# Attention and two MLP layers on one core: TensorE kept at work with zeros, and VectorE, GpSimd and ScalarE reordered in the attention stage

## The chip, the cores and the metric

The kernel runs on one core of a Trainium2 chip. The metric is the device time of one execution in microseconds (us), as the median of several runs. Engines: TensorE (PE) does matrix products, VectorE (DVE) and ScalarE (ACT) elementwise work and can read PSUM, GpSimd (POOL) elementwise work on SBUF, SyncE (SP) issues the loads.

## The reference

```
scores = q @ k^T / 8            # (4 batches, 8 heads, 576 x 576), head_dim 64
thresh = max(scores) - tau      # tau = 0.02
scores = where(scores >= thresh, scores, -1e9)
attn   = exp(scores - max) / (sum + 1e-9)
x      = attn @ v               # as (2304 tokens, 512)
h = x @ w_in;  g = s * relu(h)**2 + b;        x = g @ w_out       # d_ff 2048
h = x @ w_in2; g = h * sigmoid(1.702 * h);    out = g @ w_out2
```

## The kernel before

All products but those of the probabilities are done in three parts: an operand is split in a high part (`_hi`, rounded for the fast fp32r mode) and a low part (`_lo`, the rest), and hi x hi, hi x lo and lo x hi are added up. For scores the three parts take two products, because q and its low part lie above each other on the partitions (`q_hl`). High parts are made by ScalarE, low parts by VectorE or GpSimd.

Attention goes by tiles: 128 (or 96) queries of one head against 576 keys. Two tiles make a beat; there are 160 tiles, and 85 beats with the last pieces. Each engine has its own order, written out by hand as a loop over beats, and semaphores join them:

- TensorE: scores of the beat's two tiles into two PSUM buffers (`scores_of`; `buffer_free` waits until `mask` is through with the buffer's last tile), then for the first 32 tiles the transposes of the probabilities of tile j - 4 (`turn_tile`), then a context product, probabilities times v (`context_of`), whose result is called a piece. In beats 3 to 14 the piece is alone: 128 tokens of a pair of heads into the one PSUM bank `shared`. From beat 16 on pieces ride: 192 tokens, beside the scores in PSUM. From beat 15 on each beat also does one step of the first MLP layer (`hidden`, and `output` three steps later), s = beat - 15.
- VectorE: `row_max` (scales the scores in PSUM and takes the row maximum, through an accumulator that is read by a small instruction of its own), `limit_of` (maximum and tau), `mask` (drops exponentials under the limit and adds up the row), `invert_pair`, `context_lo` (low part of a piece, `act_lo`), `gated` and `gated_lo` (the MLP's gate and its low part `g_lo`), and from tile 32 on `turn` (32x32 transposes, in place of TensorE's).
- ScalarE: `exponent`, `context_hi` (high part of a piece, `act_hi`), `copy_main` and `copy_tails` (transposed probabilities out of PSUM), the high parts of q, k and the weight slabs.
- GpSimd: low parts of q, k (`splits`) and the slabs, `norm` (probabilities times the inverse sum), `add_eps_pair`.
- SP: loads, in order.

A piece that is alone has one bank, so the product waits for the low part of the piece before; its waits at the beat are, in order, for the copies of the transposed probabilities and then:

```
                    if piece > 0:
                        pe.wait_ge(context_lo_ready, piece)
                i = VALUE_OF[piece]
                pe.wait_ge(v_loaded[i % 2], 16 * (i // 2 + 1))
```

The first step of the MLP waits for all twelve such pieces (`context_lo_ready, LONE_PIECES`). After the attention come the rest of the first layer and then the second layer, which is done in pairs of token tiles and slabs with seven products in place of eight. Neither is touched.

Of the kernel before, what the change touches and what calls it, by code (L numbers as in the profile page):

```python
# [233 lines left out]
SPLITS_BEHIND = PE_TILES // 2 + 2  # L234

HASTY = 3 * PAIRS_PER_BATCH - 1

# [114 lines left out]
def build(nc, q, k, v, consts_in, ident_in, slabs, twin_in, twin_out, out):  # L354
    ctx = ExitStack()
    with ctx:
# [3 lines left out]
        def sbuf(stack, name, shape, dt=F32):  # L360
            return stack.enter_context(nc.sbuf_tensor(name, shape, dt))
# [74 lines left out]
        row_sum_eps = sbuf(attn, "row_sum_eps", [P, STATS])  # L436
        row_inv = sbuf(attn, "row_inv", [P, STATS])
        eps_pair = sbuf(attn, "eps_pair", [P, 2])
        attn.close()

        b_hi.insert(0, sbuf(ctx, "b_hi0", [P, PRODUCT_COUNT, 2, TOK], F32R))
# [23 lines left out]
        consts_ready = sem("consts_ready")  # L465
        lower_set = sem("lower_set")
        pads_zeroed = sem("pads_zeroed")
        table_loaded = sem("table_loaded")
        q_loaded = [sem(f"q_loaded{n}") for n in range(Q_RING)]
        k_loaded = [sem(f"k_loaded{n}") for n in range(2)]  # L470
# [139 lines left out]
        def _(sp):  # L610
# [50 lines left out]

            load_k(0)
            load_q(0)
            sp.dma_start(consts[:, 0:3], consts_in).then_inc(consts_loaded, 16)
            load_k(1)
            load_q(1)
            sp.dma_start(ident[:], ident_in).then_inc(ident_loaded, 16)
            load_q(2)
# [60 lines left out]
        def _(pe):  # L729
# [232 lines left out]
            def mlp(s):  # L962
# [4 lines left out]
                if 0 <= s < STEPS:  # L967
                    hidden(s)

            for beat in range(BEATS):  # L970
                due = turn_due(beat - MLP_FROM)
                for j in tiles_of(beat):
                    if j < TILES or (j % 2 == 0 and due is not None) or (j % 2 == 1 and riding(beat) is not None):
                        buffer_free(j)
                    if j % 2 == 0 and due is not None:
                        turn_riding(*due)
                    if j % 2 == 1 and riding(beat) is not None:
                        context_of(riding(beat))
                    if j < TILES:
                        scores_of(j)  # L980
                    if 0 <= j - 4 < PE_TILES:
                        turn_tile(j - 4)
                if alone(beat) is not None:
                    context_of(alone(beat))
                mlp(beat - MLP_FROM)
# [16 lines left out]

        @block.vector
        def _(dve):
            nc.vector.memset(lower_c[0:64, :], 0.0).then_inc(lower_set, 1)
            nc.vector.memset(lower_c[64:128, :], 1.0).then_inc(lower_set, 1)
            dve.wait_ge(consts_loaded, 16)
            nc.vector.tensor_scalar(scale_c, tau_in, 0.0, -SCALE, ALU.is_ge, ALU.mult).then_inc(consts_ready, 1)
            nc.vector.tensor_scalar(tau_c, tau_in, 0.0, None, ALU.max).then_inc(consts_ready, 1)
            dve.wait_ge(k_hi_ready, 1)  # L1010
            nc.vector.tensor_tensor(k_lo[key_slot(0)][:], k_raw[key_slot(0)][:], k_hi[key_slot(0)][:].bitcast(F32),
                                    ALU.subtract).then_inc(k_lo_ready, 1)
            dve.wait_ge(q_hi_ready, 1)
            nc.vector.tensor_tensor(q_hl[0][:, 0:q_width(0)], q_raw[:, 0, 0:q_width(0)],
                                    q_hl[0][:, 0:q_width(0)].bitcast(F32), ALU.subtract
                                    ).then_inc(q_lo_ready, 1)
            dve.wait_ge(consts_ready, 2)

            def row_max(j):
# [6 lines left out]
                                        accum_out=neg_max[0:m, j % STATS:j % STATS + 1]  # L1026
                                        ).then_inc(max_ready, 1)

            def limit_of(j):
                m, r = rows_of(j), j % STATS  # L1030
                dve.wait_ge(max_ready, j + 1)
                nc.vector.tensor_scalar(limit[0:m, r:r + 1], neg_max[0:m, r:r + 1], tau_c[0:m, :], None, ALU.add  # L1032
                                        ).then_inc(limit_ready, 1)

            def invert_pair(j):
# [5 lines left out]
            def mask(j):  # L1041

                m, r = rows_of(j), j % STATS
                dve.wait_ge(limit_ready, j + 1)
                dve.wait_ge(exp_ready, j + 1)
                if j % 2 == 1 and riding(j // 2) is not None:
                    dve.wait_ge(context_hi_ready, riding(j // 2) + 1)
                if j % 2 == 0 and turn_due(j // 2 - MLP_FROM) is not None:
                    dve.wait_ge(x_ready, turns_by(j // 2 - MLP_FROM))
                p = prob[0:m, j % PROBS, :].rearrange("p (a n) -> p a n", a=2)  # L1050
                nc.vector.scalar_tensor_tensor(  # L1051
                    out=p, in0=scores[j % 2][0:m, :, 0:HALF], scalar=limit[0:m, r:r + 1],
                    in1=p, op0=ALU.is_le, op1=ALU.mult,
                    accum_out=row_sum[0:m, r:r + 1]).then_inc(masked, 1)
# [101 lines left out]
            def low_block(d, i):  # L1156
# [2 lines left out]
                nc.vector.tensor_tensor(g2_lo[:, i, :], gate2[:, i % 2, :], g2_hi[:, i, :].bitcast(F32),  # L1159
                                        ALU.subtract).then_inc(g2_lo_ready, 1)  # L1160

            for beat in range(BEATS):
                s = beat - MLP_FROM
                for j in tiles_of(beat):
                    if j < TILES:
                        row_max(j)
                        limit_of(j)
                    if j % 2 == 0 and alone(beat - 1) is not None:
                        context_lo(alone(beat - 1))
                    if j % 2 == 0 and 0 <= j - 2 < TILES:  # L1170
                        invert_pair(j - 2)
                    if j % 2 == 0 and s >= 1:
                        gated(s - 1)
                for j in tiles_of(beat):
                    if j < TILES:
                        mask(j)
                    if j % 2 == 0 and s >= 2:
                        gated_lo(s - 2)
                if riding(beat) is not None:
                    context_lo(riding(beat))  # L1180
                for j in tiles_of(beat, 2):
                    if PE_TILES <= j < TILES:
                        turn(j)
# [39 lines left out]
        def _(act_eng):  # L1223
# [180 lines left out]
            for beat in range(BEATS):  # L1404
                s = beat - MLP_FROM
                if alone(beat - 1) is not None:
                    context_hi(alone(beat - 1))
                for j in tiles_of(beat):
                    if j < TILES:
                        exponent(j)  # L1410
                    if j % 2 == 0 and 0 <= j - 4 < PE_TILES:
                        copy_tails(j - 4)
                    if j % 2 == 0 and turn_due(s) is not None:
                        x_riding(s)
                for j in tiles_of(beat, 4):
                    if 0 <= j < PE_TILES:
                        copy_main(j)
                if riding(beat) is not None:
                    context_hi(riding(beat))
                if tile_ends(s - 1) and s + 1 < STEPS:  # L1420
                    slab_in_hi(s + 1)
                if s >= 1:
                    gated_hi(s - 1)
                if tile_ends(s):
                    copy_rows(s - OUT_LAG)
                    if s < STEPS:
                        gate_of(s)
                if s >= 1:
                    slab_out_hi(s - 1)
                for i in range(2, len(Q_LOADS)):  # L1430
                    if q_split_beat(i) == beat:
                        split_q(i)
                for e in range(2, HEADS):
                    if key_split_beat(e) == beat:
                        split_k(e)
                if not tile_ends(s):
                    if 0 <= s < STEPS:
                        gate_of(s)
                    if 0 <= s + 2 < STEPS:
                        slab_in_hi(s + 2)  # L1440
# [58 lines left out]
        def _(pool):  # L1499
# [14 lines left out]
            def split_k(e):  # L1514

                pool.wait_ge(k_hi_ready, e + 1)
                if e == 1:
                    pool.wait_ge(k_lo_ready, 1)
                nc.gpsimd.tensor_tensor(k_lo[key_slot(e)][:], k_raw[key_slot(e)][:], k_hi[key_slot(e)][:].bitcast(F32),
                                        ALU.subtract).then_inc(k_lo_ready, 1)  # L1520

# [25 lines left out]
                                        wout_hi[n % OUT_HI][:].bitcast(F32), ALU.subtract  # L1547
                                        ).then_inc(wout_lo_ready, 1)

            def splits(beat):  # L1550
                for i in range(2, len(Q_LOADS)):
                    if q_split_beat(i) + 1 == beat:
                        split_q(i)
                for e in range(2, HEADS):
                    if key_split_beat(e) + 1 == beat:
                        split_k(e)

            pool.wait_ge(pads_zeroed, 2)
            split_k(1)
            split_q(1)  # L1560
            for beat in range(BEATS):
                s = beat - MLP_FROM
                if s >= 2:
                    slab_out_lo(s - 2)
                if beat < SPLITS_BEHIND:
                    splits(beat)
                for j in tiles_of(beat, 2):
                    if 0 <= j < TILES:
                        norm(j)
                if s >= 2:  # L1570
                    pool.wait_ge(g_lo_ready, s - 1)
                if beat >= SPLITS_BEHIND:
# [105 lines left out]
```

## Time and profile before

| | |
|---|---|
| median of 3 runs | 1013.93 us (1013.07 to 1015.03) |
| profiled execution | 1013.14 us |
| its span | 1011.3 us |
| PE busy | 988.5 us (98%) |
| DVE busy | 796.9 us (79%) |
| ACT busy | 606.3 us (60%) |
| POOL busy | 658.3 us (65%) |

The span runs from the first to the last instruction; the execution's own time has 1.84 us more around it. Matmul ends are modelled, so that PE's busy share says little about its rate; where PE stands idle and what ended the wait is to be read from the timeline and the waits. Attention ends near 484 us.

### The profile page before, as it was taken

To read this page: it belongs to the slowest core of one execution; us is meant where nothing else is said; L and a number is where in the kernel's file an instruction comes from. 1 tells how busy PE (TensorE), PEld (TensorE's weight loads), DVE (VectorE), ACT (ScalarE), POOL (GpSimd) and SP (SyncE) were. 2 spreads that over 40 slices of the span, in tenths; PEclk is the share of its full clock that TensorE was granted. 3 is DMA by queue.
4 is the path that set the end of the run, shared out by engine and by line. 5 is a ranking of instruction groups with operands and counts; after the bars stand their busy time and mean duration, and the time that the engine had idled before them with its cause. 6 is when DMAs were issued, how large, how long until landed. Compare 5 with 4: busy or idle time off the path is not lost.

```text
span 1011.3 us, 18111 instructions
## 1 busy us (share of the span) xinstructions
PE 988.5 (98%) x5872; PEld 890.6 (88%) x5872; DVE 796.9 (79%) x1747; ACT 606.3 (60%) x1124; POOL 658.3 (65%) x714
## 2 busy tenths in 40 slices
PE   5999999999999999999999999999999999999998
PEld 4888888888888888888899999998898989898897
DVE  6999999999999999999646765877667777556663
ACT  5887666666576666665545756554546545454453
POOL 5768997778888788887657775444534544445442
PEclk9999999999999999999999999999999999999999
DMA  6235776788777888678733441112122321222212
GB/s 205 82 99 168 204 207 208 193 242 237 211 192 196 225 218 222 191 185 214 207 122 126 172 162 34 41 64 84 42 84 71 118 84 43 83 82 106 84 47 78
DMA packets 97580, 142.48 MB, mean 141 GB/s; under 512 B 10320, under 2 KB 68944, under 8 KB 97488
## 3 DMA queue, kind: packets, MB, share of 16 engines
q1 hardware_dynamic: 97488, 141.34, 47.8%
q8 instruction: 48, 0.79, 0.3%
q14 instruction: 44, 0.36, 0.1%
HBM read 102.96 MB, written 4.72 MB: 106 GB/s over the span
## 4 chain that ended last, share of the span: by engine, by line
PE 87%; DVE 10%; issue 1%; ACT 1%; DMA 0%; POOL 0%; SPq 0%; DVEq 0%; POOLq 0%; ACTq 0%
PE shared L825 12%; PE y_ps L844 11%; PE shared L918 10%; PE y_ps L942 10%; PE scores L942 10%; PE scores L918 8%; PE scores L739 8%; PE scores L801 7%; PE scores L825 5%; PE y_ps L864 5%; DVE scores L1025 4%; DVE prob L1051 3%; PE scores L864 2%; DVE blocks L1065 1%; DVE limit L1032 1%
## 5 line engine op out<-in xcount | busy, mean ns | idle before, releaser
L1248 ACT ACTIVATE prob<-scores,neg_max 128x576 f32<-128x576 f32 (+1 forms) x160 | 118.6, 741 | 126.1 <-DVE scores L1025 124.0
L1590 POOL TENSOR_TENSOR a_sum_lo<-a_sum,a_hi 128x256 fp32r<-128x256 f32 x96 | 70.1, 740 | 182.7 <-DVE scores L1147 124.0
L1025 DVE TENSOR_SCALAR_CACHE_REDUCE scores<-scores,consts 128x576 f32<-128x576 f32 (+1 forms) x160 | 129.5, 809 | 18.1 <-PE scores L739 16.6
L1539 POOL TENSOR_TENSOR w_lo<-w_raw,win_hi 128x512 fp32r<-128x512 f32 x96 | 129.0, 1344 | 22.1 <-ACT win_hi L1290 17.7
L1546 POOL TENSOR_TENSOR w_lo<-w_raw,wout_hi 128x512 fp32r<-128x512 f32 x96 | 126.4, 1316 | 23.6 <-ACT wout_hi L1297 23.5
L1533 POOL TENSOR_SCALAR prob<-prob,row_inv 128x576 f32<-128x576 f32 (+1 forms) x160 | 126.5, 803 | 5.5 <-DVE row_inv L1039 5.0
L1051 DVE SCALAR_TENSOR_TENSOR prob<-scores,limit,prob 128x576 f32<-128x576 f32 (+1 forms) x160 | 128.1, 808 | 0.9 <-ACT act_hi L1258 0.9
L825 PE MATMUL shared<-act_hi,win_hi 128*128 128x384 f32 x280 | 94.9, 339 | 1.1 <-DVE gate L1081 0.9
L825 PE MATMUL shared<-act_hi,w_lo 128*128 128x384 f32 x280 | 94.4, 337 | 0.0
L739 PE MATMUL scores<-k_hi,q_hl 128*128 128x288 f32 (+1 forms) x320 | 78.0, 326 | 16.8 <-DVE prob L1051 9.0
L825 PE MATMUL shared<-act_lo,win_hi 128*128 128x384 f32 x280 | 94.0, 336 | 0.0
L1088 DVE SCALAR_TENSOR_TENSOR g_lo<-gate,consts,g_hi 128x384 fp32r<-128x384 f32 x96 | 92.6, 964 | 0.2 <-ACT g_hi L1311 0.2
L1065 DVE STREAM_TRANSPOSE blocks<-prob 128x576 f32<-128x576 f32 (+1 forms) x128 | 91.4, 751 | 1.3 <-DMA prob_t<-blocks 1.1
L1159 DVE TENSOR_TENSOR g_lo<-gate,g_hi 128x384 fp32r<-128x384 f32 x96 | 62.2, 650 | 33.4 <-ACT g_hi L1382 32.8
L1311 ACT ACTIVATE g_hi<-gate,consts 128x384 fp32r<-128x384 f32 x96 | 59.0, 615 | 38.8 <-PE y_ps L864 28.0
L1374 ACT ACTIVATE gate<-scores 128x384 f32<-128x384 f32 x48 | 23.6, 491 | 94.9 <-DVE scores L1147 94.9
L1382 ACT CAST g_hi<-gate 128x384 fp32r<-128x384 f32 x96 | 49.2, 515 | 49.4 <-DVE gate L1154 40.0
L739 PEld LDWEIGHTS scores<-k_hi,q_hl 128*128 128x128 f32 (+1 forms) x320 | 49.9, 183 | 32.3 <-DVE prob L1051 14.3
L844 PE MATMUL y_ps<-wout_hi,g_hi 128*128 128x512 f32 x192 | 75.6, 394 | 0.0
L844 PE MATMUL y_ps<-wout_hi,g_lo 128*128 128x512 f32 x192 | 75.5, 393 | 0.0
L801 PE MATMUL scores<-prob_t,v_sb 128*64 128x192 f32 x800 | 73.9, 331 | 1.2 <-DVE prob L1051 0.9
L844 PE MATMUL y_ps<-w_lo,g_hi 128*128 128x512 f32 x192 | 74.9, 390 | 0.0
(154 smaller groups left out, 2945.1 us busy)
## 6 DMA issues: line engine op xcount, KB each, us to landing
w_raw<-slabs SPq DMA_DIRECT2D x93, 512.0 KB, 4.1
a_raw<-twin_in SPq DMA_DIRECT2D x24, 512.0 KB, 4.5
o_raw<-twin_out SPq DMA_DIRECT2D x24, 512.0 KB, 3.5
prob_t<-blocks SPq DMA_DIRECT2D x96, 120.0 KB, 2.7
k_raw<-k SPq DMA_DIRECT2D x32, 288.0 KB, 4.2
prob_t<-blocks SPq DMA_DIRECT2D x96, 96.0 KB, 2.9
v_sb<-v SPq DMA_DIRECT2D x26, 320.0 KB, 4.3
q_raw<-q SPq DMA_DIRECT2D x40, 192.0 KB, 4.4
```

What stands on the lines that cost most here:

```text
L739: mm = nc.tensor.matmul(scores[j % 2][0:m, half, 0:HALF], q_hl[i % Q_RING][:, q0:q0 + m], part[key_slot(e)][:, half * HALF:(half + 1) * HALF],
L801: mm = nc.tensor.matmul(place, v_sb[:, i % 2, side, c, :], rows, start=(c == 0), stop=(c == KEY_CHUNKS - 1))
L825: mm = nc.tensor.matmul(bank[:, 0:TOK], wp[:, w], act_at(xp, c, tile * TOK, TOK), start=(c == 0 and k == 0), stop=(c == DC - 1 and k == 2))
L844: mm = nc.tensor.matmul(y_ps[g][:], gp[:, n % 2, toks], wp[:, :], start=(f == 0 and k == 0), stop=(f == SLABS - 1 and k == 2))
L918: mm = nc.tensor.matmul(twin_bank(x), wp, xp, start=(c == 0 and k == 0), stop=(c == 1 and k == 2))
L942: mm = nc.tensor.matmul(z_bank(tile, g), gp[:, i, toks], wp, start=(e == 0 and i < 2 and k == 0), stop=(e == TWIN_SLABS - 1 and i >= 2 and ...
L1025: nc.vector.tensor_scalar(place, place, scale_c[0:m, :], None, ALU.mult, ALU.min, accum_out=neg_max[0:m, j % STATS:j % STATS + 1]).then_in ...
L1051: nc.vector.scalar_tensor_tensor(out=p, in0=scores[j % 2][0:m, :, 0:HALF], scalar=limit[0:m, r:r + 1], in1=p, op0=ALU.is_le, op1=ALU.mult, ...
L1248: nc.scalar.activation(prob[0:m, j % PROBS, :].rearrange("p (a n) -> p a n", a=2), scores[j % 2][0:m, :, 0:HALF], ACT.Exp, bias=neg_max[0: ...
L1533: nc.gpsimd.tensor_scalar(prob[0:m, j % PROBS, :], prob[0:m, j % PROBS, :], row_inv[0:m, r:r + 1], 1.0, ALU.mult, ALU.mult).then_inc(norme ...
L1539: nc.gpsimd.tensor_tensor(in_of(w_lo, n), in_of(w_raw, n), win_hi[n % IN_HI][:].bitcast(F32), ALU.subtract).then_inc(win_lo_ready, 1)
L1546: nc.gpsimd.tensor_tensor(out_of(w_lo, n), out_of(w_raw, n), wout_hi[n % OUT_HI][:].bitcast(F32), ALU.subtract).then_inc(wout_lo_ready, 1)
```

## The change

Five edits. The order of TensorE gets products of zeros that nobody reads: ten ahead of the first scores, eight behind the scores of tile 1, seven behind those of tile 3, into the unused columns of a PSUM bank. VectorE does head 1's low part instead of GpSimd, and its constants after the first low parts; SP loads head 1's keys ahead of the constants. VectorE takes the limits of a beat's two tiles in one operation, behind `context_lo` and `gated_lo`, which now stand ahead of both masks. ScalarE does `context_hi` of a riding piece ahead of `copy_main`. GpSimd, in beat 1, splits only load 2 ahead of the norms and the rest behind them.

```diff
+AWAKE_FIRST = 10
+AWAKE = (0, 8, 0, 7)
...
+        zeros = sbuf(attn, "zeros", [P, P])
...
             load_q(0)
+            load_k(1)
             sp.dma_start(consts[:, 0:3], consts_in).then_inc(consts_loaded, 16)
-            load_k(1)
...
+            def keep_awake(n):
+                for _ in range(n):
+                    nc.tensor.matmul(y_ps[2][:, 2 * P:3 * P], zeros[:], zeros[:], start=True, stop=True)
+
+            pe.wait_ge(zeros_set, 1)
+            keep_awake(AWAKE_FIRST)
...
                     if j < TILES:
                         scores_of(j)
+                    if j < len(AWAKE):
+                        keep_awake(AWAKE[j])
...
         def _(dve):
+            nc.vector.memset(zeros[:], 0.0).then_inc(zeros_set, 1)
...
-            dve.wait_ge(consts_loaded, 16)
-            nc.vector.tensor_scalar(scale_c, tau_in, 0.0, -SCALE, ALU.is_ge, ALU.mult).then_inc(consts_ready, 1)
-            nc.vector.tensor_scalar(tau_c, tau_in, 0.0, None, ALU.max).then_inc(consts_ready, 1)
...
+            split_k(0)
             dve.wait_ge(q_hi_ready, 1)
...
+            dve.wait_ge(consts_loaded, 16)
+            nc.vector.tensor_scalar(scale_c, tau_in, 0.0, -SCALE, ALU.is_ge, ALU.mult).then_inc(consts_ready, 1)
+            nc.vector.tensor_scalar(tau_c, tau_in, 0.0, None, ALU.max).then_inc(consts_ready, 1)
             dve.wait_ge(consts_ready, 2)
...
+                dve.wait_ge(max_ready, j + 2)
+                nc.vector.tensor_scalar(limit[0:m, r:r + 2], neg_max[0:m, r:r + 2], tau_c[0:m, :], None, ALU.add
                                         ).then_inc(limit_ready, 1)
...
+            split_k(1)
             for beat in range(BEATS):
                 s = beat - MLP_FROM
                 for j in tiles_of(beat):
                     if j < TILES:
                         row_max(j)
-                        limit_of(j)
-                    if j % 2 == 0 and alone(beat - 1) is not None:
-                        context_lo(alone(beat - 1))
                     if j % 2 == 0 and 0 <= j - 2 < TILES:
                         invert_pair(j - 2)
                     if j % 2 == 0 and s >= 1:
                         gated(s - 1)
+                if alone(beat - 1) is not None:
+                    context_lo(alone(beat - 1))
+                if s >= 2:
+                    gated_lo(s - 2)
+                if 2 * beat < TILES:
+                    limit_pair(2 * beat)
                 for j in tiles_of(beat):
                     if j < TILES:
                         mask(j)
-                    if j % 2 == 0 and s >= 2:
-                        gated_lo(s - 2)
...
+                if riding(beat) is not None:
+                    context_hi(riding(beat))
                 for j in tiles_of(beat, 4):
                     if 0 <= j < PE_TILES:
                         copy_main(j)
-                if riding(beat) is not None:
-                    context_hi(riding(beat))
...
-            split_k(1)
             split_q(1)
...
-                if beat < SPLITS_BEHIND:
+                if beat == 1:
+                    split_q(2)
+                elif beat < SPLITS_BEHIND:
                     splits(beat)
                 for j in tiles_of(beat, 2):
                     if 0 <= j < TILES:
                         norm(j)
+                if beat == 1:
+                    splits(beat, 3)
```

## Rows read from the trace of the kernel before

**Rows 1.** Page, the chain that ended last, by engine.
```profile
PE 87%; DVE 10%; issue 1%; ACT 1%; DMA 0%; POOL 0%; SPq 0%; DVEq 0%; POOLq 0%; ACTq 0%
```
**Rows 2.** Busy time by window: PE, PEld, DVE, ACT, POOL, clock, DMA share, GB/s.
```profile
150.00:200.00 50.00, 49.81 (x317) 43.62 (x314) 47.77 (x122) 32.15 (x60) 36.70 (x44) 1.00 0.73 199
```
**Rows 3.** Timeline, 0 to 22 us: start, duration, instruction, idle before and releaser.
```profile
4.58 0.15 DVE L1008 TENSOR_SCALAR consts<-consts 128x1 f32<-128x1 f32 x1 [3.62 <-DMA consts<-consts_in]
...
5.84 0.85 PE L739 MATMUL scores<-k_hi,q_hl 128*128 128x288 f32 x2 [5.84 <-DVE q_hl L1014]
6.00 0.67 ACT L1238 CAST k_hi<-k_raw 128x576 fp32r<-128x576 f32 x1 [1.26 <-DMA k_raw<-k]
...
6.82 1.40 POOL L1519 TENSOR_TENSOR k_lo<-k_raw,k_hi 128x576 fp32r<-128x576 f32 x1 [4.50 <-ACT k_hi L1238]
...
8.36 0.82 PE L739 MATMUL scores<-k_hi,q_hl 128*128 128x288 f32 x2 [1.18 <-POOL k_lo L1519]
...
11.62 0.85 PE L739 MATMUL scores<-k_hi,q_hl 128*128 128x288 f32 x2 [1.96 <-DVE prob L1051]
...
16.00 0.85 PE L739 MATMUL scores<-k_hi,q_hl 128*128 128x288 f32 x2 [2.10 <-DVE prob L1051]
...
21.32 0.53 PE L739 MATMUL scores<-k_hi,q_hl 128*128 128x288 f32 x2 [1.32 <-DVE prob L1051]
```
**Rows 4.** Timeline, one beat of the stage with attention alone.
```profile
29.23 0.53 PE L739 MATMUL scores<-k_hi,q_hl 128*128 128x288 f32 x2 [0.32 <-DVE prob L1051]
...
30.67 0.42 PE L739 MATMUL scores<-k_lo,q_hl 128*128 128x288 f32 x2
...
31.11 0.28 DVE L1073 TENSOR_TENSOR act_lo<-shared,act_hi 128x128 fp32r<-128x128 f32 x1
...
31.38 0.81 DVE L1025 TENSOR_SCALAR_CACHE_REDUCE scores<-scores,consts 128x576 f32<-128x576 f32 x1
...
31.64 1.31 PE L801 MATMUL shared<-prob_t,v_sb 128*64 128x128 f32 x20
...
32.10 0.14 DVE L1025 DVE_READ_ACCUMULATOR scores<-scores,consts 128x1 f32 x1
...
32.41 0.81 DVE L1051 SCALAR_TENSOR_TENSOR prob<-scores,limit,prob 128x576 f32<-128x576 f32 x1
...
33.28 0.53 PE L739 MATMUL scores<-k_hi,q_hl 128*128 128x288 f32 x2 [0.33 <-DVE prob L1051]
```
**Rows 5.** Timeline, 68 to 77 us: context products, and the first MLP product.
```profile
68.10 1.31 PE L801 MATMUL shared<-early_t,v_sb 128*64 128x128 f32 x20 [0.33 <-DVE act_lo L1073]
...
69.73 0.50 PE L739 MATMUL scores<-k_hi,q_hl 128*96 128x288 f32 x2 [0.32 <-DVE prob L1051]
...
71.98 0.19 PEld L825 LDWEIGHTS shared<-act_hi,win_hi 128*128 128x128 f32 x1 [0.34 <-POOL w_lo L1539]
...
75.21 1.84 PE L801 MATMUL scores<-prob_t,v_sb 128*64 128x192 f32 x20
...
76.98 0.51 PE L739 MATMUL scores<-k_hi,q_hl 128*96 128x288 f32 x2
```
**Rows 6.** Waits of PE, 75 to 125 us (total, times, longest); beat 16's timeline.
```profile
PE shared L825 <- DVE gate L1081: 0.9, 3, 0.5
PE scores L801 <- DVE prob L1051: 0.9, 2, 0.5
PE scores L739 <- DVE act_lo L1073: 0.5, 1, 0.5
...
79.35 0.84 ACT L1269 COPY prob_t<-y_ps 128x384 f32<-128x384 f32 x2
...
80.53 0.81 DVE L1051 SCALAR_TENSOR_TENSOR prob<-scores,limit,prob 96x576 f32<-96x576 f32 x1 [0.88 <-ACT act_hi L1258]
```
**Rows 7.** Timeline near 97 us; groups of 150 to 480 us (busy, mean ns).
```profile
96.64 2.09 POOL L1533 TENSOR_SCALAR prob<-prob,row_inv 96x576 f32<-96x576 f32 x2
...
97.17 0.94 DVE L1088 SCALAR_TENSOR_TENSOR g_lo<-gate,consts,g_hi 128x384 fp32r<-128x384 f32 x1
...
L1088 DVE SCALAR_TENSOR_TENSOR g_lo<-gate,consts,g_hi 128x384 fp32r<-128x384 f32 x51 | 34.8, 682 | 0.0
```

More of the change, by code:

```diff
@@ L467, in build @@
         pads_zeroed = sem("pads_zeroed")
+        zeros_set = sem("zeros_set")
         table_loaded = sem("table_loaded")
@@ L1004, in _, with split_k @@
         def _(dve):
+            nc.vector.memset(zeros[:], 0.0).then_inc(zeros_set, 1)
             nc.vector.memset(lower_c[0:64, :], 0.0).then_inc(lower_set, 1)
             nc.vector.memset(lower_c[64:128, :], 1.0).then_inc(lower_set, 1)
-            dve.wait_ge(consts_loaded, 16)
-            nc.vector.tensor_scalar(scale_c, tau_in, 0.0, -SCALE, ALU.is_ge, ALU.mult).then_inc(consts_ready, 1)
-            nc.vector.tensor_scalar(tau_c, tau_in, 0.0, None, ALU.max).then_inc(consts_ready, 1)
-            dve.wait_ge(k_hi_ready, 1)
-            nc.vector.tensor_tensor(k_lo[key_slot(0)][:], k_raw[key_slot(0)][:], k_hi[key_slot(0)][:].bitcast(F32),
-                                    ALU.subtract).then_inc(k_lo_ready, 1)
+            def split_k(e):
+                dve.wait_ge(k_hi_ready, e + 1)
+                nc.vector.tensor_tensor(k_lo[key_slot(e)][:], k_raw[key_slot(e)][:], k_hi[key_slot(e)][:].bitcast(F32),
+                                        ALU.subtract).then_inc(k_lo_ready, 1)
+            split_k(0)
             dve.wait_ge(q_hi_ready, 1)
@@ L1027, in row_max, with limit_pair @@
                                         ).then_inc(max_ready, 1)
-            def limit_of(j):
+            def limit_pair(j):
                 m, r = rows_of(j), j % STATS
-                dve.wait_ge(max_ready, j + 1)
-                nc.vector.tensor_scalar(limit[0:m, r:r + 1], neg_max[0:m, r:r + 1], tau_c[0:m, :], None, ALU.add
+                dve.wait_ge(max_ready, j + 2)
+                nc.vector.tensor_scalar(limit[0:m, r:r + 2], neg_max[0:m, r:r + 2], tau_c[0:m, :], None, ALU.add
                                         ).then_inc(limit_ready, 1)
@@ L1043, in mask @@
                 m, r = rows_of(j), j % STATS
-                dve.wait_ge(limit_ready, j + 1)
+                dve.wait_ge(limit_ready, j // 2 + 1)
                 dve.wait_ge(exp_ready, j + 1)
@@ L1516, in split_k @@
                 pool.wait_ge(k_hi_ready, e + 1)
-                if e == 1:
-                    pool.wait_ge(k_lo_ready, 1)
+                if e == 2:
+                    pool.wait_ge(k_lo_ready, 2)
                 nc.gpsimd.tensor_tensor(k_lo[key_slot(e)][:], k_raw[key_slot(e)][:], k_hi[key_slot(e)][:].bitcast(F32),
@@ L1548, in slab_out_lo, with splits @@
                                         ).then_inc(wout_lo_ready, 1)
-            def splits(beat):
-                for i in range(2, len(Q_LOADS)):
+            def splits(beat, first=2):
+                for i in range(first, len(Q_LOADS)):
                     if q_split_beat(i) + 1 == beat:
```

## The prediction

> **What bounds the kernel now.** I read the chain that ended last first [rows 1]: TensorE has 87% of it, VectorE 10%. The 50 us windows of the middle [rows 2] show where each has its share: there TensorE is busy all the time at a granted clock of 1.00, and VectorE 47.77 of 50 us, so TensorE bounds it and VectorE is close behind. From there to the end TensorE waits for nothing of size, so the time is decided before about 112 us: whatever the changed kernel has won or lost by then arrives at the end as it is. Next I read the timeline of the first 22 us [rows 3], one beat in the stage with attention alone [rows 4], the moments where the context product or the first MLP step waits [rows 5], and TensorE's waits from 75 to 125 us [rows 6].
>
> The start is a chain of single waits: the first score matmul begins at 5.84, the second head's at 8.36 (after GpSimd's k_lo, 6.82 plus 1.40), tile 2 at 11.62, tile 4 at 16.00, tile 6 at 21.32. A pair of 128x288 matmuls takes 0.85 us up to 16.00 and 0.53 at 21.32 [rows 3], so that TensorE runs at its lower level of 1.2 GHz until it has worked nearly without a break from 16.00 on. The clock column says 1.00 in both, so I go by durations.
>
> In the stage with attention alone a beat of two tiles takes 33.28 - 29.23 = 4.05 us [rows 4], and its last link is VectorE's first mask (start 32.41, then 0.87 to the next scores).
>
> **The change, part by part.** Times are against the profiled execution (1013.14 us, span 1011.3 and 1.84 around it); the median shown, 1013.93, is 0.8 higher.
>
> *Start, beats 0 to 2.* VectorE no longer waits 3.62 us for the constants before k_lo. k_hi(0) ends near 4.34, so k_lo(0) runs 4.4 to 5.05, q_lo to 5.5, and scores start at 5.55 instead of 5.84. The key load of head 1 is issued one place (0.48 us) earlier; its conversion, which had waited for the load until 6.00, starts near 5.7 and ends at 6.4. The constants come behind it on SP's queue, near 6.0, which two operations of 0.15 us after q_lo absorb. Then VectorE does k_lo(1) 6.45 to 7.2, at 0.75 for what GpSimd did in 1.40. Its first row maximum starts right behind, 7.1 against 7.32, so it lies in nobody's way, and scores(1) can start at 7.25 instead of 8.36.
> The zeros: one fp32 matmul of 128 columns. The nearest rows are the context products, five slots (two halves side by side) of 128 columns in 1.31 us [rows 4] and of 192 in 1.84 [rows 5]: 0.53/(5 x 64) = 1.66 ns a column, 0.21 to 0.26 us for 128, twice that at the lower clock. The memset is one small operation (GpSimd's 64x768 took 0.73; 0.1 to 0.3 here). So ten zeros run from about 1 us to 5.3 (half of them fast) or 6.0 (all slow). Bounds: nothing, or 0.5 us of delay to scores(0), of which VectorE's k_lo(1) hides most. I take 0. If TensorE is fast by 7 us, scores(1) ends at 8.05, its row maximum at 9.0, the common limit at 9.05, mask(0) starts at 9.2, and scores(2) start at 10.05: 1.55 gained. The eight zeros behind scores(1) take 8 x 0.25 = 2.0 and end at 10.05 as well, so they cost nothing, with no margin. Beat 1 took 4.38; two score groups at the faster pair time (0.3 us less a pair, one group in the chain: 0.5) and one limit (0.13 plus the gap before it) less make 3.65; seven zeros end 0.4 before the next scores. Beat 2 took 5.32 with slow transposes in its chain; I work out 4.1: scores 0.8, row maximum, a wait of about 0.4 for the inverse, row maximum, 1.0 to the mask, 0.87. That wait is new: GpSimd now does norm(0) and norm(1) before the splits of load 3 and head 2 (0.73 + 1.40), and the addition of eps, on which VectorE's next reciprocal waits, stands behind them. Gain at tile 6: 1.55 + 0.73 + 1.22 = 3.5, and 3.4 a beat later, since GpSimd's norm(2) is 0.2 late. Bounds 2.4 to 4.3.
>
> *Beats 4 to 14.* Here the change adds a wait. The context product of a beat waits for act_lo of the piece before (one bank), and act_lo moves from ahead of the second row maximum to behind it. Queued behind the product on TensorE are the next beat's scores. Before, act_lo ends at 31.39 and the product starts at 31.64, 0.25 later [rows 4]; at 68.10 TensorE even waited for act_lo by name, 0.33 us [rows 5]. So it was on the edge already. Now, counted from a beat's first scores: second scores end at 30.67 + 0.42 - 29.23 = 1.86, row maximum from 1.90, its accumulator read at 2.62 (0.72 later, as 31.38 to 32.10), act_lo 2.68 to 2.96, product from 3.21. How soon the next scores can follow: the 192-column product began at 75.21 and scores at 76.98, 1.77 against a duration of 1.84, so 0.07 less than the duration; for 128 columns 1.31 - 0.07 = 1.24. Next beat: 3.21 + 1.24 = 4.45, or 4.42 with the weight load's lead; I take 4.43. The mask path, which loses a limit of 0.13, would allow 3.95, 0.10 under today. So each beat is 0.38 longer: eleven beats, +4.2. Bounds: act_lo could start with the accumulator read (4.37) or 0.17 after it (4.54), the order in which it waits for other things adding nothing: +3.4 to +5.2.
>
> *Beat 15.* The first MLP product needs act_lo of the last piece. Today it starts at 71.98, 2.25 after the beat's scores at 69.73 (they follow the product of 68.10 by 1.63), released by GpSimd. With act_lo ending at 2.8 it starts near 3.0: +0.75 (0.4 to 0.9).
>
> *75 to 112 us.* TensorE's waits there, 0.9 + 0.9 + 0.5 = 2.3 us [rows 6], are the most that this stage can give. At beat 16 the mask at 80.53 had waited 0.88 for the conversion of the piece, which ScalarE did behind two copies from 79.35 (0.84); "piece first" starts that mask near 79.7, 0.83 earlier, and frees 1.0 of TensorE's waits. What moves behind the piece is a copy that the transposes need a beat later; nothing waits. For the rest VectorE must be faster. It loses a limit of 0.13 and two gaps, 0.34 a beat together, but g_lo now runs before both masks. Today g_lo takes 0.61 alone and 0.94 at 97.17, under GpSimd's two norms, which took 2.09 instead of 1.47 [rows 7]: one blocked the other. The new place of g_lo is 1.4 us after the reciprocal that releases the norms, and the norms last 1.47 plus 0.25 of start: a block of about 0.3 in most beats, where the middle of the kernel now has 0.682 - 0.61 = 0.07 on average. So VectorE gains next to nothing a beat. I take -1.4 of the 2.3 (bounds -0.8 and -2.0).
> The Trainium skill states the same as a rule ("SBUF — State Buffer", Who interferes with whom): a VectorE operation with two SBUF inputs and a GpSimd operation that reads SBUF hold one port pair in turn, and the later one waits for the whole of the other. By it g_lo's block would be the rest of the running norm, up to a whole one, 0.75 on GpSimd, not a share of both; the 0.94 here agrees. It speaks against this move, and is the third rival below.
>
> Sum: -3.4 + 4.2 + 0.75 - 1.4 = +0.15 us, so 1013.3 in the terms of the profiled execution and about 1014.0 as a median. No change that can be told: a measurement of this kernel tells 0.2%, 2 us.
>
> **The rivals.**
> *The act_lo wait stays hidden.* Then beats 4 to 14 gain the 0.10 of the limit each (-1.1), beat 15 costs nothing, and the sum is -3.4 - 1.1 - 1.4 = -5.9: 1008.0. For it: the product usually starts just as the transposes end, so today's start does not prove a wait. Against it: 68.10, and in my working the order leaves act_lo no place before 2.6.
> *The zeros run slow.* If zeros don't raise the clock before scores(1), these end at 8.6, eight zeros last 8 x 0.5 = 4.0, and tile 2 starts at 12.6 instead of 11.62. Compared with my 10.05 that is 2.5 us: 1016.5, slower than before. If the seven of beat 1 are slow too, tile 4 starts at 18.4 and the loss is 4.6: 1018.6. It decides as soon as a zero costs over 0.3 us at 8 us. For it: nothing in the trace shows what zeros do to the clock. Against: the rise came about 3 us after the work that began at 16.00, and ten zeros are over 4 us of unbroken work.
> *g_lo against the norms makes VectorE the bound.* VectorE has 50 - 47.77 = 2.2 us in 50 to spare, 0.28 a beat of 6.3 us. With 0.34 won, it is decided from a block of 0.62 a beat on. At 0.70 it costs 0.08 in each of 66 beats, 5 us: 1019. Against: the norms are through, or nearly, when g_lo starts.
>
> **How the numbers follow.** Forecast 0.66, own range 1011.8 to 1016.2 from the bounds above, not all at one end; the hidden wait 0.14; slow zeros 0.10; the blocked g_lo 0.10. The first rival and its 0.14 stay below the range, the far end of the third above it: 1010 to 1018. Faster (below 1011.9): 0.14 and 0.10 of the forecast's. Slower (above 1016.0): 0.18 of the rivals and 0.10. Within: 0.46 and 0.02.
>
> **What would show it.** Tile 6's scores near 17.8; pairs of 0.53 us from about 7 us on; beats 4 to 14 at 4.43 with TensorE waiting for act_lo at each context product; the first MLP product 3.0 after its beat's scores; that is, near 73.5; no wait of 0.88 at beat 16; g_lo at 0.9 in most beats and no TensorE wait after 112 us. Wrong, if beats 4 to 14 take 3.95, or the zeros hold up tile 2, or TensorE waits for masks in the middle.

## The result, and the profile after

The changed kernel takes 1038.67 us (median of 6 runs, 1037.76 to 1043.1) against 1014.36 for the kernel before in the same measurement: a ratio of 1.0244 (95% interval 1.0229 to 1.026), 24 us slower, where the prediction said 1014.0 and at most 1018. The profiled execution's span is 1036.0 us, 24.7 longer than before.

First the page's chain that ended last, which before had 87% for PE and 10% for DVE [rows 1].

```profile
PE 78%; DVE 12%; issue 3%; DMA 3%; SPq 2%; ACT 1%; POOL 0%; DVEq 0%; POOLq 0%; ACTq 0%
```

The 3% of DMA and 2% of SPq are new as well; without the pair (e1 below) each is 1%.

Next the windows of the changed kernel, columns as in [rows 2].

```profile
100.00:150.00 50.00, 42.79 (x230) 36.05 (x229) 48.91 (x93) 28.57 (x51) 39.36 (x40) 0.93 0.59 163
150.00:200.00 50.00, 48.34 (x301) 41.59 (x300) 48.98 (x111) 28.89 (x52) 39.28 (x44) 1.00 0.68 187
...
126.00:130.00 4.00, 2.30 (x12) 1.75 (x11) 3.96 (x8) 1.00 (x2) 2.30 (x3) 0.88 0.24 91
130.00:134.00 4.00, 4.00 (x16) 3.35 (x15) 3.96 (x10) 1.96 (x3) 3.43 (x4) 0.69 0.35 74
```

TensorE stands idle for 7 of the 50 us from 100 to 150 and for 1.7 in the 50 that [rows 2] show as full, while VectorE is busy. Here the granted clock falls below 1.00, to means of 0.88 and 0.69 in the two stretches shown (and to 0.89 and 0.68 from 102 to 110): a part of each at 1.2 GHz. TensorE had stood idle for 1.7 of the 4 us from 126 to 130.

To see where the time goes I compared the starts of the first row maximum of each beat in the two traces (difference in us, after minus before):

```
beat     3      4      9     15     16     18     20     22     26     40     60     79
      -3.15  -2.93  -0.92  +1.24  +1.84  +1.56  +5.70  +8.55 +13.52 +15.85 +20.38 +23.83
```

The start won 3.2 us, beats 4 to 14 gave 4.2 back, both as forecast. From beat 18 on the kernel loses 22 us: 12 of them by beat 26, 14.4 by beat 28 (+15.92), then nothing up to beat 40 and 8 more by the end of attention. Behind attention nothing more is lost that matters (24.7 at the end).

The start, in the timeline of the changed kernel:

```profile
1.05 4.63 PE L978 MATMUL y_ps<-zeros 128*128 128x128 f32 x20 [1.05 <-DVE zeros L1019]
...
5.56 0.79 PE L745 MATMUL scores<-k_hi,q_hl 128*128 128x288 f32 x2
...
5.67 0.76 DVE L1026 TENSOR_TENSOR k_lo<-k_raw,k_hi 128x576 fp32r<-128x576 f32 x1
...
6.19 0.43 PE L745 MATMUL scores<-k_lo,q_hl 128*128 128x288 f32 x2
...
9.46 0.53 PE L745 MATMUL scores<-k_hi,q_hl 128*128 128x288 f32 x2 [0.34 <-DVE prob L1072]
...
14.19 0.54 PE L745 MATMUL scores<-k_hi,q_hl 128*128 128x288 f32 x2 [1.63 <-DVE prob L1072]
...
18.17 0.54 PE L745 MATMUL scores<-k_hi,q_hl 128*128 128x288 f32 x2 [1.56 <-DVE prob L1072]
```

Ten products of zeros take 4.63 us, 0.46 each, and from 6.19 on pairs are fast. Tile 6's scores start at 18.17 instead of 21.32 [rows 3].

Beat 4, and the first MLP product:

```profile
22.27 0.53 PE L745 MATMUL scores<-k_hi,q_hl 128*128 128x288 f32 x2 [0.43 <-DVE prob L1072]
...
25.46 1.31 PE L807 MATMUL shared<-prob_t,v_sb 128*64 128x128 f32 x20 [0.78 <-DVE act_lo L1094]
...
26.70 0.52 PE L745 MATMUL scores<-k_hi,q_hl 128*128 128x288 f32 x2
...
70.97 0.50 PE L745 MATMUL scores<-k_hi,q_hl 128*96 128x288 f32 x2
...
73.85 0.41 PE L831 MATMUL shared<-act_hi,win_hi 128*128 128x384 f32 x1 [0.75 <-POOL w_lo L1562]
```

The context product now waits for act_lo, starts 3.19 after the scores, and the next scores follow 1.24 behind it: 4.43 us a beat against 4.05 [rows 4].

Then the place of the loss, one beat of the mixed stage, from the timelines of VectorE, GpSimd and TensorE:

```profile
99.48 2.08 POOL L1556 TENSOR_SCALAR prob<-prob,row_inv 96x576 f32<-96x576 f32 x2
...
100.30 0.64 DVE L1109 SCALAR_TENSOR_TENSOR g_lo<-gate,consts,g_hi 128x384 fp32r<-128x384 f32 x1
100.86 2.09 DVE L1053 TENSOR_SCALAR limit<-neg_max,consts 96x2 f32<-96x2 f32 x1
...
101.52 1.41 POOL L1542 TENSOR_TENSOR k_lo<-k_raw,k_hi 128x576 fp32r<-128x576 f32 x1
...
102.99 0.81 DVE L1072 SCALAR_TENSOR_TENSOR prob<-scores,limit,prob 96x576 f32<-96x576 f32 x1
...
103.87 0.51 PE L745 MATMUL scores<-k_hi,q_hl 128*96 128x288 f32 x2 [1.75 <-DVE prob L1072]
```

The operation that makes the two limits, two numbers a partition, takes 2.09 us. It starts while GpSimd does a norm, is not through when GpSimd goes on with k_lo at 101.52, and ends at 102.95, just as k_lo does (102.93). The mask starts behind it, and TensorE's next scores wait 1.75 us for the mask. The limits' group over the stage, and g_lo's (columns as in [rows 7]; before, g_lo 682 ns from 150 to 480 us):

```profile
L1053 DVE TENSOR_SCALAR limit<-neg_max,consts 128x2 f32<-128x2 f32 (+1 forms) x59 | 49.1, 832 | 0.0
L1109 DVE SCALAR_TENSOR_TENSOR g_lo<-gate,consts,g_hi 128x384 fp32r<-128x384 f32 x58 | 42.4, 731 | 0.0
```

The 59 operations of 75 to 480 us take 832 ns on average (215 to 3082 over the kernel). One column took 0.21 us each before. The timelines show that this is no exception: of the 78 such operations that start before 500 us, 49 take over 0.3 us, and 47 of these end within 0.05 us of the end of a row of GpSimd's (the other two end inside a row that joins two norms); the other 29 take 0.21 to 0.25. TensorE's waits over the whole kernel, total, times, longest:

```profile
PE scores L745 <- DVE prob L1072: 15.4, 16, 2.0
PE shared L807 <- DVE act_lo L1094: 8.8, 11, 0.9
```

### The profile page after: what moved, and what is told of

Read it like the earlier page. It is cut to its first block, busy times and chain, and to the rows that moved or that the text cites. A ratio compares the mean times of both kernels' runs of the same rounds, so it can differ in the third digit from the quotient of the medians.

```text
span 1036.0 us, 18132 instructions
## 1 busy us (share of the span) xinstructions
PE 1002.1 (97%) x5922; PEld 895.9 (86%) x5922; DVE 820.4 (79%) x1669; ACT 608.6 (59%) x1124; POOL 672.1 (65%) x713
## 4 chain that ended last, share of the span: by engine, by line
PE 78%; DVE 12%; issue 3%; DMA 3%; SPq 2%; ACT 1%; POOL 0%; DVEq 0%; POOLq 0%; ACTq 0%
PE shared L924 9%; PE y_ps L948 9%; PE scores L948 9%; PE shared L831 9%; PE y_ps L850 8%; PE scores L924 7%; PE scores L745 7%; PE scores L807 6%; PE scores L831 5%; PE y_ps L870 5%; DVE scores L1045 4%; DVE limit L1053 3%; DVE blocks L1086 2%; DVE prob L1072 2%; PE scores L870 2%
## 5 line engine op out<-in xcount | busy, mean ns | idle before, releaser
L1556 POOL TENSOR_SCALAR prob<-prob,row_inv 128x576 f32<-128x576 f32 (+1 forms) x160 | 140.8, 892 | 4.3 <-DVE row_inv L1060 3.8
L1072 DVE SCALAR_TENSOR_TENSOR prob<-scores,limit,prob 128x576 f32<-128x576 f32 (+1 forms) x160 | 124.4, 814 | 3.9 <-ACT prob L1271 1.1
L1109 DVE SCALAR_TENSOR_TENSOR g_lo<-gate,consts,g_hi 128x384 fp32r<-128x384 f32 x96 | 95.5, 995 | 0.2 <-ACT g_hi L1334 0.2
L745 PEld LDWEIGHTS scores<-k_hi,q_hl 128*128 128x128 f32 (+1 forms) x320 | 47.3, 179 | 38.2 <-DVE prob L1072 25.2
```

The lines of the kernel that those rows point to most:

```text
L745: mm = nc.tensor.matmul(scores[j % 2][0:m, half, 0:HALF], q_hl[i % Q_RING][:, q0:q0 + m], part[key_slot(e)][:, half * HALF:(half + 1) * HALF],
L1072: nc.vector.scalar_tensor_tensor(out=p, in0=scores[j % 2][0:m, :, 0:HALF], scalar=limit[0:m, r:r + 1], in1=p, op0=ALU.is_le, op1=ALU.mult, ...
L1556: nc.gpsimd.tensor_scalar(prob[0:m, j % PROBS, :], prob[0:m, j % PROBS, :], row_inv[0:m, r:r + 1], 1.0, ALU.mult, ALU.mult).then_inc(norme ...
```

## The experiments

Theory A: an operation on two columns cannot run while GpSimd works, and one column can. Rival B: g_lo's new place makes the masks late. Eleven kernels ran, in three groups, each group beside the kernel before on one chip: e1 to e5 (before 1014.09 us), e6 to e9 (1013.66) and e10 to e13 (1013.92). Ratios are against the kernel before of the same group. Differences between kernels of different groups, or against the 1038.67, are those of the medians; since the kernel before itself moved by up to 0.7 us between these measurements, they are uncertain by as much.

**e1, limits one by one.** In the changed kernel (shortened; each mask then waits for its own tile's limit):

```diff
-                nc.vector.tensor_scalar(limit[0:m, r:r + 2], neg_max[0:m, r:r + 2], ...).then_inc(limit_ready, 1)
+                for n in range(r, r + 2):
+                    nc.vector.tensor_scalar(limit[0:m, n:n + 1], neg_max[0:m, n:n + 1], ...).then_inc(limit_ready, 1)
```

> The changed kernel, but the two limits of a beat are two operations of one column each, at the same place behind g_lo. Theory A (the one operation on two columns cannot run while GpSimd works, and waits for norms and splits): the limits take 0.21 us each again and the time falls from 1038.7 to 1013 to 1017. Rival B (the loss comes from g_lo, moved ahead of both masks): the time stays above 1030 and g_lo or the masks show the waits.

Measured 1012.34 us, ratio 0.9984 (0.9973 to 0.9994). Its groups of 75 to 480 us:

```profile
L1110 DVE SCALAR_TENSOR_TENSOR g_lo<-gate,consts,g_hi 128x384 fp32r<-128x384 f32 x62 | 46.1, 743 | 0.0
L1054 DVE TENSOR_SCALAR limit<-neg_max,consts 128x1 f32<-128x1 f32 (+1 forms) x126 | 20.4, 200 | 0.0
```

This one edit takes 26.3 us off, a little more than A said. g_lo is where it was and takes as long (743 ns), so B is refuted.

**e2, the pair alone.** The kernel before, with `limit_pair` behind the second row maximum and nothing else changed; g_lo stays between the masks.

> The kernel before, with one thing changed: the limits of two tiles in one operation of two columns, behind the second row maximum and ahead of the first mask; g_lo stays between the masks. Theory A: the operation takes over 0.5 us on average from 75 us on, since the norms run then, and the kernel is slower than before, 1018 to 1035. Rival B: 0.2 us an operation, 1011 to 1014.

Measured 1022.17, ratio 1.0076 (1.0055 to 1.0098).

```profile
L1032 DVE TENSOR_SCALAR limit<-neg_max,consts 128x2 f32<-128x2 f32 (+1 forms) x63 | 31.2, 495 | 2.2
```

495 ns a pair, just under the half microsecond expected, and 8 us lost. So the pair makes even the old order slower, but a third as much as in the changed kernel. In its trace 3.3 of 7.9 us are lost by beat 15, with beats 4 to 14 at 4.26 us, and the operations it waits for are not norms alone but GpSimd's w_lo too.

**e4, splits held back.** The rest may come from the splits, which g_lo lets go just ahead of the pair in the new order. On GpSimd:

```diff
                     pool.wait_ge(g_lo_ready, s - 1)
+                    if 2 * beat < TILES:
+                        pool.wait_ge(limit_ready, beat + 1)
```

> The changed kernel, but GpSimd's splits wait for the limits as well as for g_lo, so that no split is let go between g_lo and the limits. Theory A: the two-column operation then waits for the running norm only, its mean falls from 0.83 to about 0.5 us, and the time comes out between 1018 and 1030. Rival B: no change, 1037 to 1040.

Measured 1021.17, ratio 1.0064 (1.0046 to 1.0082).

```profile
L1053 DVE TENSOR_SCALAR limit<-neg_max,consts 128x2 f32<-128x2 f32 (+1 forms) x61 | 31.6, 518 | 0.0
```

A wait added on GpSimd makes the kernel 17.5 us faster, and no pair takes over 0.83 us now. What is left, 8.8 us over e1, is the pair behind the norms.

**e5, act_lo back, pair kept.** `context_lo(alone(beat - 1))` goes back ahead of the second row maximum.

> The changed kernel, but VectorE does act_lo of a lone piece at its old place, ahead of the second row maximum. If the wait of the context product for act_lo is what makes beats 4 to 14 4.43 us long, they take 3.9 to 4.05 and attention's second stage begins 4 to 5.5 us earlier; the whole time then falls by 3 to 5 us, to 1034 to 1036. Rival: these beats are long for another reason (limits, copies) and stay over 4.3.

Measured 1037.16, ratio 1.0223 (1.0203 to 1.0243): 1.5 us off, not 3 to 5. The beats became 4.27 us long instead of 4.43 (from the row maxima of beats 4 and 15). The timeline of one:

```profile
45.96 1.31 PE L807 MATMUL shared<-prob_t,v_sb 128*64 128x128 f32 x20
...
46.44 0.69 DVE L1053 TENSOR_SCALAR limit<-neg_max,consts 128x2 f32<-128x2 f32 x1
...
48.05 0.53 PE L745 MATMUL scores<-k_hi,q_hl 128*128 128x288 f32 x2 [0.78 <-DVE prob L1072]
```

The product no longer waits, but the pair takes 0.69 under the norms, and the scores wait for the mask. Two waits lay side by side, and one hid the other.

**e7, both mended.** Single limits and act_lo back:

```diff
+                    if j % 2 == 0 and alone(beat - 1) is not None:
+                        context_lo(alone(beat - 1))
                     if j % 2 == 0 and 0 <= j - 2 < TILES:
                         invert_pair(j - 2)
...
-                if alone(beat - 1) is not None:
-                    context_lo(alone(beat - 1))
```

> Single limits as in e1, and act_lo of a lone piece back ahead of the second row maximum. If act_lo's place alone makes beats 4 to 14 4.43 us long, they take 3.95 to 4.05 now, beat 15 starts 4 to 5 us earlier than in e1, and the time is 1007 to 1009. Rival: they stay near 4.27, as with the two-column limits, and the time is 1010.5 to 1011.

Measured 1006.85, ratio 0.993 (0.9917 to 0.9944), just under the range expected: 6.8 us faster than the kernel before and 5.5 faster than e1.

```profile
26.00 0.53 PE L745 MATMUL scores<-k_hi,q_hl 128*128 128x288 f32 x2 [0.40 <-DVE prob L1073]
...
28.34 1.31 PE L807 MATMUL shared<-prob_t,v_sb 128*64 128x128 f32 x20
...
29.96 0.53 PE L745 MATMUL scores<-k_hi,q_hl 128*128 128x288 f32 x2 [0.30 <-DVE prob L1073]
```

A beat takes 3.96 here, and 3.99 on average from beat 4 to 15. Beat 15 comes 5.2 us earlier than in e1.

**e8, g_lo back between the masks, on top of e7.**

> As e7, and g_lo back between the masks. If g_lo ahead of the masks collides with the norms and costs VectorE what the paired order saves, this is 0 to 2 us faster than e7, g_lo's mean from 75 to 480 us falls from 0.74 towards 0.63 us, and the masks come sooner. Rival: g_lo's place is worth nothing once TensorE is the bound: same as e7 within 0.5 us.

Measured 1007.66, ratio 0.9936 (0.9924 to 0.9947).

```profile
L1110 DVE SCALAR_TENSOR_TENSOR g_lo<-gate,consts,g_hi 128x384 fp32r<-128x384 f32 x62 | 41.6, 671 | 0.0
```

g_lo is shorter, 671 ns for e7's 742, and the kernel is 0.8 us slower all the same, with intervals that overlap; in the traces the row maximum of beat 79 comes 2.4 us later than in e7, but the profiled execution of e7 was its fastest (1006.06) and that of e8 its slowest (1008.19), so part of this is scatter. My expectation was wrong: the new place of g_lo does no harm.

**e9, the copies first again, on top of e7** (`context_hi` of a riding piece behind `copy_main`).

> As e7, but ScalarE does the conversion of a riding piece behind the copies again, as before. Forecast of the prediction for this edit: the second mask of beat 16 waits 0.8 us longer and TensorE loses about 1.0 us: 1.0 us slower than e7. Rival: it is made up by the next beats: no difference.

Measured 1007.19, ratio 0.9931 (0.9916 to 0.9945). In the traces the second mask of beat 16 waits 0.76 us, the row maximum of beat 18 comes 1.2 us later than in e7 and that of beat 79 1.0, as forecast; the medians differ by 0.3, less than either kernel's scatter, and don't tell it apart.

**e6, e1 without any zeros** (`AWAKE_FIRST = 0`, `AWAKE = (0, 0, 0, 0)`).

> The kernel with single limits (e1), without any product of zeros. If the zeros raise the clock, as the pairs of 0.53 us from 6.2 us on suggest, the pairs take 0.85 us again until about 18 us, tile 6's row maximum comes 1.0 to 2.0 us later than with zeros (near 20 to 21), and the time is 1013 to 1014.5. Rival: the start is bound by loads and masks, and the zeros save nothing: same as e1 within 0.5 us.

Measured 1014.95, ratio 1.0009 (1.0 to 1.0017): 2.6 us slower than e1, a little over the range expected. Pairs take 0.82 to 0.85 us up to 22.57, longer than the expected 18, and 0.53 at 25.97. The row maximum of tile 6 comes at 21.89 instead of 18.93. So of the 3.2 us that the start wins in e1, the zeros are 3.0, and the other edits of the start together little by then (tile 2's row maximum is 0.9 earlier than before, but later tiles lose that again).

**e13, the first ten zeros only, on top of e7** (`AWAKE = (0, 0, 0, 0)`).

> e7 with the ten zeros ahead of the first scores, but without the eight and the seven later ones. If the ten are enough, the pairs stay at 0.53 us through the first 20 us and the time is e7's, 1006.5 to 1007.5. If the clock falls in TensorE's waits of about 2 us in beats 0 to 2, the pairs go back to 0.85 us and the time is 1008 to 1009.5.

Measured 1008.88, ratio 0.9949 (0.9933 to 0.9966): 2.0 slower than e7.

```profile
5.58 0.57 PE L745 MATMUL scores<-k_hi,q_hl 128*128 128x288 f32 x2
...
7.27 0.50 PE L745 MATMUL scores<-k_hi,q_hl 128*128 128x288 f32 x2 [0.85 <-DVE k_lo L1026]
...
10.12 0.85 PE L745 MATMUL scores<-k_hi,q_hl 128*128 128x288 f32 x2 [2.09 <-DVE prob L1073]
```

The clock rises and falls again: 0.50 us a pair at 7.27, and 0.85 at 10.12, after TensorE had stood idle for 0.85 and 2.09 us. The later zeros are what keeps it. The windows of e13 (columns as in [rows 2]; the clock is third from the end) show the fall and the return as well:

```profile
8.00:10.00 2.00, 0.03 (x1) 0.00 (x0) 1.89 (x7) 1.75 (x3) 0.00 (x0) 0.78 0.68 192
10.00:12.00 2.00, 1.88 (x8) 1.88 (x8) 1.32 (x5) 1.20 (x3) 0.88 (x2) 0.50 0.61 225
...
20.00:22.00 2.00, 2.00 (x16) 1.96 (x17) 1.76 (x6) 2.00 (x5) 0.80 (x2) 1.00 0.90 344
```

**e10 and e11, a spare operation.** To e7, ahead of the limits and read by nobody, in e10 with two columns and in e11 with one (`0:1`):

```diff
+                nc.vector.tensor_scalar(spare[0:m, 0:2], zeros[0:m, 0:2], tau_c[0:m, :], None, ALU.add)
                 for n in range(r, r + 2):
```

> The fast version e7 (single limits, act_lo back) with one small operation more a beat ahead of the limits: it adds a constant to two columns of zeros in SBUF and writes them to a spare tile, and nothing waits for it. Theory A (two columns alone make an operation wait for GpSimd): the operation takes 0.5 to 0.9 us on average and up to 3 us, and the time rises from 1006.9 to 1020 to 1035. Rival (only the dependence of the limits on the row maxima made the long operation): 0.2 us, 1007 to 1009.

> The same with one column instead of two. Theory A: 0.13 to 0.21 us each, hidden behind TensorE but for the beats ahead of 112 us: 1007 to 1009.5. Rival (any further operation at this place costs the same): as e10.

e10 took 1042.4, ratio 1.028 (1.0264 to 1.0295), 35.6 us more than e7 and above the range expected; e11 took 1010.39, ratio 0.9967 (0.9954 to 0.998), 3.5 more and somewhat over the range expected. The group of e10, then that of e11, 75 to 480 us:

```profile
L1054 DVE TENSOR_SCALAR spare<-zeros,consts 128x2 f32<-128x2 f32 (+1 forms) x59 | 48.0, 813 | 0.1
```

```profile
L1054 DVE TENSOR_SCALAR spare<-zeros,consts 128x1 f32<-128x1 f32 (+1 forms) x63 | 12.7, 202 | 0.0
```

One operation, at one place, on zeros, with nothing that depends on it: 202 ns with one column, 813 with two (up to 3074; with one column never over 215). That settles A against every reading by dependence or place.

## Why the prediction was wrong

**The step that failed** is in "75 to 112 us": VectorE "loses a limit of 0.13 and two gaps, 0.34 a beat together". The prediction priced the new operation like half of what it replaces, from the duration of the one-column form, and never asked whether a second column changes what it waits for. It measured 0.83 us on average, 0.22 at its shortest, and up to 3.08. The average hides where the loss falls. From beat 28 on the operation takes 0.62 us on average, 0.40 more than when nothing holds it: that uses up the 0.34 forecast as a gain, and VectorE's spare 0.28 a beat mostly takes the rest. In beats 18 to 27 it takes 1.91, 1.69 too much; less the 0.34 and the 0.28 this leaves about 1.1 us a beat, 11 us in ten beats (an estimate from these rows), where the kernel lost 14.4. e1 shows the size of the whole: 26.3 us. Because the operation was given no bound from above, the range could not hold the result.

The Trainium skill has the rule, in the very section that the prediction drew on for g_lo ("SBUF — State Buffer", Who interferes with whom): `tensor_scalar` without an accumulator output can enter a two-port mode, which contends with GpSimd for the shared port pair. "VectorE: DVE Perf Modes", Mode 2×_2P, adds the condition: the operands lie in SBUF, and the access pattern is split in half along its outermost non-unit dimension. By that a single column cannot be split and two can. The runs agree on both sides, 202 against 813 ns; that it is the two ports and not something else about two columns, they do not show. No run has a form that reads its two columns from PSUM, which could tell.

**Why so much in the changed order.** g_lo ends just ahead of the pair, and its end lets GpSimd start the next split. In the beat shown the pair missed the gap between two GpSimd operations and waited for the second one as well. Holding the splits back (e4) gave 17.5 us, so this overlap was two thirds of the loss; the pair under the norms is the rest, 8.8 us (e4 less e1). That e2 also lost 8 us is partly chance: 3.3 of them come before beat 15, where e4 is only 0.4 behind e1. Why VectorE does not get in between the two operations of GpSimd is open. TensorE's clock added a part: after waits of up to 2 us it was down for some stretches (mean 0.997 over the span of 1036 us, so at most about 3 us in all, an estimate).

**The start: right.** Forecast -3.4, measured -3.15 at tile 6 and -2.93 at beat 4. TensorE was fast from about 6 us on, which the rival of the slow zeros denied, and e6 and e13 show that the zeros made it so. That the sum fits so well is partly luck, since two errors cancel in it. Tile 2's scores came at 9.46, 2.16 earlier than before where 1.55 was forecast: head 1's keys were converted from 4.76 on, not from 5.7. Beat 1 then took 4.73 us and not 3.65: its first mask (13.31) waited 1.07 us for an exponential, ScalarE having waited 1.42 for the keys of head 2 (converted at 11.89), which I had left out. Beat 2 took 3.98 for 4.1, but without the wait of 0.4 us for the inverse that I had put there: the reciprocal at 15.77 follows the row maximum at once, and nowhere in the trace does VectorE wait for the sum that it needs. The zeros ahead of the scores took 4.63 us, all at the lower clock, for 5.0 forecast; the other end given there, 5.3 us for half of them fast, was mis-added (from 1 us on, five of 0.5 and five of 0.25 end at 4.8).

**Beats 4 to 14: right, to the hundredth.** Forecast 4.43 us; measured 48.68/11 = 4.43, with the product 3.19 behind the beat's scores for 3.21. It waits for act_lo eleven times, 8.8 us in all. The other path, through the mask, was put at 3.95; with the pair it takes 4.27 (e5), with single limits at most 3.99 (e7). The rival of the hidden wait is refuted, by the row and by e7. What act_lo's place costs is 5.5 us with single limits, and only 1.5 with the pair.

**Beat 15: right in size.** The product came 2.88 after the scores, forecast 3.0, though by the profile GpSimd's w_lo released it; but w_lo had ended at 73.11, and act_lo ended at 73.74, 0.1 before the product.

**Piece first: borne out by one pair of traces** (1.2 us at beat 18 in e9), below what the medians tell.

**75 to 112 us otherwise.** e1 shows the stage without the pair: from +1.9 at beat 16 to -1.2 at beat 24, 3.1 us against 1.4 forecast, out of the same waits [rows 6] and some that came later. The term was sized too small because I gave g_lo a block of about 0.3 us in most beats (0.9 us for 0.61). In e1 it takes 0.743 on average, 0.13 over the 0.61, and its place was a gain: of the 3.0 us that e7 wins from beat 16 to 24, 1.3 are gone in e8's trace, with g_lo between the masks, and 1.1 in e9's, with the copies first (one trace each).

**The third rival** named the right resource and the wrong operation. g_lo took 731 ns in the changed kernel against 696 before over the same stretch, and moving it back (e8) gained nothing.

So the sum of 1014.0, which has the pair at its forecast price, stands beside e1's 1012.34; what the changed kernel takes beyond e1 is the one term.

## What to carry to other kernels

Merging two small VectorE operations into one can change what they wait for: here one column more made an operation of 0.2 us wait for GpSimd, up to 3 us, on the chain to TensorE. Before merging, see what GpSimd does at that moment; two one-column operations took 0.32 us together and did not wait for it (e1). And when a semaphore that lets another engine go is moved, ask what that engine will start, and beside which instruction. Where two waits end close together, undo both: putting act_lo back gave 1.5 us beside the pair (e5) and 5.5 beside single limits (e7 less e1), and both together made the fastest kernel, 1006.85 us.

## What the runs showed of the hardware that I had not expected

A VectorE operation on 128x2 numbers in SBUF took 215 to 3082 ns depending on what GpSimd was doing; on 128x1 numbers at the same place 198 to 215 (e11).

TensorE at work on zeros, whose products nobody reads, runs fast later: the first pair of 128x288 matmuls of a group took 0.57 us at 5.58 and 0.50 at 7.27, after 4.6 us of unbroken zeros, and 0.85 again at 10.12 when the zeros between were left out (e13). The clock column of the windows says 1.00 until the first fall, although durations show the lower level (0.46 us a product of zeros in the first 5 us of the changed kernel; pairs of 0.85 up to 16.00 in the kernel before [rows 3]). From the first fall on it agrees with the durations: 0.78 and then 0.50 in e13 from 8 to 18 us, 0.68 and 0.69 in stretches between 102 and 134 us of the changed kernel. So in these traces a 1.00 ahead of the first fall doesn't show the level; durations do.
